# A bias table's relu tiles spread over VectorE, GpSimd and ScalarE, with its log table in PSUM and its output copies on two engines

## The chip, the core and the metric

One core of one Trainium2 chip runs the kernel. Its engines are TensorE (PE, with its weight loads as PEld), VectorE (DVE), ScalarE (ACT), GpSimd (POOL) and SyncE (SP), which here only issues DMAs. The metric is device time in microseconds, the median of several runs. VectorE and ScalarE reach PSUM as well as SBUF; TensorE writes its products to PSUM.

## The reference

```python
def _attn_ref(q, k, v, w1, b1, w2):          # q, k, v: (4, 8, 576, 64); hidden = 32
    scores = scale * np.matmul(q, k.transpose(0, 1, 3, 2))
    rel = (pos[:, None] - pos[None, :]).astype(np.float32)
    psi_rel = np.log1p(np.abs(rel))
    psi_i = np.log1p(np.maximum(pos[:, None].astype(np.float32), 1.0))
    x = (psi_rel / psi_i)[..., None]
    h = np.maximum(x @ w1 + b1, 0.0)
    bias = h @ w2                             # (576, 576, 8): one table for all batches
    scores = scores + bias.transpose(2, 0, 1)[None, :, :, :]
    attn = softmax(scores)
    return np.matmul(attn, v)

# layer 1: x = max(x@w1, x@w2, x@w3) @ w_out      # 2304 tokens, 512 -> 768 -> 512
# layer 2: out = g(x @ w_in) @ w_out                         # 512 -> 2048 -> 512
```

## The kernel before

The kernel has four stages one after the other: the bias table, attention (32 pairs of batch and head), and the two feed-forward layers. Each engine runs its own list of instructions in order and waits on semaphores for the others. The change touches the first stage only.

**The bias table.** `log_t` [128, 1148] holds log(1 + |n|) for every distance n, shifted per partition: partition p = 32 r + c belongs to row r of a group of four query rows and to hidden unit c. `row_sc` holds, per partition and group, w1 divided by the log of the query position. A *group* is four rows (G4 = 4), a *super-tile* (here: a bias tile) is four groups or 16 rows, and NSUP = 36 bias tiles make 576 rows. They are worked on in rounds of four: i is the round (0 to 8), j or e the place in it (0 to 3).

For bias tile s four relu tiles [128, 576] are made, g = 0 to 3: each is relu(log_t shifted by s and g, times row_sc, plus b1). g = 0 to 2 are made by VectorE (`hidden`, line 768) as max(x * row_sc, -b1), which is the relu less b1; g = 3 by ScalarE (`hidden_act`, line 571). The constant that is missing is computed once (`nconst`, line 585) and added at the copy. The relu tiles lie in `hid[e]`, four buffers in the memory of xT. TensorE multiplies each by `w2b` (`bias_tile`, line 941): 8 matmul calls, 16 instructions, into the two PSUM banks 2e and 2e+1, so four bias tiles fill the eight banks. ScalarE copies the two banks to `bias_o[:, e]` in SBUF (`bias_copy`, line 578), and SyncE stores it to `bias_scratch` in DRAM (`store_bias`, line 371).

**The waits.** A relu tile waits until the bias tile four before it has been multiplied (`bias_ps`). `bias_tile` waits for its relu tiles (`hid_ok`, `hid_act`) and for the copy of the bias tile four before (`bias_sb`). A copy waits for its bias tile and for `bias_free[e]`, which the store of four tiles before raises; for the first four it is raised by SyncE itself (line 367) after it has issued the loads of q, k and v for the first two heads (lines 330 to 352). On ScalarE the order is relu s, copy s-2, relu s+1, copy s-1 and so on.

**Around it.** GpSimd makes the initial tables and zeroes, then two `dup`s of q and k (line 493), and then waits for attention. SyncE loads the first head's bias back from DRAM in pieces (`load_first_bias`, line 376): 864 KB after the stores of round 6 are issued, 144 KB after those of round 7, the rest once all stores have landed, followed by line 396 (its tail) and by the second head's bias. TensorE's first transposes of attention (line 968) wait for all copies, since they use the same banks. The first step of attention on VectorE (line 811) waits for the first head's bias.

## Time and profile before

| | |
|---|---|
| time, median of 3 runs | 1166.76 us (1163.58 to 1167.42) |
| span of the profiled execution | 1165.9 us |
| what lies around the span, against the median | 0.9 us |
| TensorE busy | 1110.3 us, 95% |
| VectorE busy | 661.2 us, 57% |
| ScalarE busy | 592.9 us, 51% |
| GpSimd busy | 323.9 us, 28% |
| bias table: first relu to end of last copy | 6.4 to 63.3 us |

The page gives busy time over the whole span. The stages have different limits, so the stage of a change has to be read by itself, from the start and end of single instructions. An instruction's duration may overlap the next one's on the same engine, so the distance from start to start (the pitch) is given where it counts. Times in rows are microseconds from the start of the span, unless marked ns.

### The profile page before, as it was taken

The numbers are of one execution on the slowest core, as the hardware profiler recorded it, in microseconds if no ns is written. First come the engines' busy times: TensorE is split into PE (matmuls) and PEld (weight loads), VectorE is DVE, ScalarE is ACT, GpSimd is POOL, SyncE is SP. The second block draws the span as 40 slices with busy tenths as digits, with TensorE's granted clock in tenths as the row PEclk, the third lists the DMA queues.
The fourth block names the chain that finished last, engine by engine and source line by source line (L and its number), as shares of the span: only waits on it lengthen the run. The fifth ranks groups of instructions, "written<-read, shape, count | busy, mean of one in ns | idle before, by whom it ended". The sixth has DMA issues, their size and how long they took to land.

```text
span 1165.9 us, 21224 instructions
## 1 busy us (share of the span) xinstructions
PE 1110.3 (95%) x6872; PEld 1013.0 (87%) x6872; DVE 661.2 (57%) x1441; ACT 592.9 (51%) x1226; POOL 323.9 (28%) x463
## 2 busy tenths in 40 slices
PE   6878999999999989999999999799999999999998
PEld 2358999999999979999999999777898998989997
DVE  8958888888888952323132222577544444444443
ACT  7957888888888863312121121344434344343433
POOL 4026767767767745300000000344000000000000
PEclk9979999999999999999999999899999999999999
DMA  3651141141141014200000000132000000000000
GB/s 133 215 176 36 42 132 41 41 132 41 41 132 41 21 36 144 74 1 1 0 0 0 0 0 1 55 109 91 28 1 27 0 0 27 0 27 0 28 1 28
DMA packets 68197, 55.29 MB, mean 47 GB/s; under 512 B 28224, under 2 KB 53824, under 8 KB 68160
## 3 DMA queue, kind: packets, MB, share of 16 engines
q1 hardware_dynamic: 68160, 54.81, 15.1%
q8 instruction: 21, 0.34, 0.1%
q14 instruction: 16, 0.13, 0.0%
HBM read 39.46 MB, written 15.34 MB: 47 GB/s over the span
## 4 chain that ended last, share of the span: by engine, by line
PE 80%; DVE 6%; ACT 3%; issue 3%; POOL 0%; ACTq 0%; DVEq 0%
PE ps L1088 34%; PE ps L1133 15%; PE ps L981 11%; PE ps L1036 6%; PE ps L1100 6%; PE ps L1048 5%; DVE tb L906 3%; ACT w_hi L664 1%; DVE s_sb L811 1%; PE ps L968 1%; PE ps L1064 1%; ACT tb L726 1%; PE ps L1072 1%; DVE x_lo L853 1%; ACT ta L720 1%
## 5 line engine op out<-in xcount | busy, mean ns | idle before, releaser
L1088 PE MATMUL ps<-x_hi,w_hi 128*128 128x384 f32 x816 | 277.5, 340 | 16.1 <-POOL w_lo L552 5.8
L1088 PE MATMUL ps<-x_hi,w_lo 128*128 128x384 f32 x816 | 275.5, 338 | 0.0
L1088 PE MATMUL ps<-x_lo,w_hi 128*128 128x384 f32 x816 | 275.3, 337 | 0.0
L1088 PEld LDWEIGHTS ps<-x_hi,w_hi 128*128 128x128 f32 x816 | 154.8, 190 | 26.8 <-POOL w_lo L552 11.8
L1088 PEld LDWEIGHTS ps<-x_lo,w_hi 128*128 128x128 f32 x816 | 154.8, 190 | 3.3
L552 POOL TENSOR_TENSOR w_lo<-raw,w_hi 128x1024 fp32r<-128x1024 f32 x27 | 64.9, 2407 | 324.4 <-ACT w_hi L664 324.2
L1088 PEld LDWEIGHTS ps<-x_hi,w_lo 128*128 128x128 f32 x816 | 154.6, 189 | 0.0
L811 DVE CUSTOM_DVE_ANT_0 s_sb<-ps,bias_h 128x576 f32<-128x576 f32 (+1 forms) x160 | 120.3, 752 | 40.7 <-PE ps L1036 30.4
L502 POOL TENSOR_SCALAR probs<-probs,row_inv 128x512 f32<-128x512 f32 (+1 forms) x160 | 108.4, 693 | 103.4 <-DVE row_inv L785 103.4
L623 ACT ACTIVATE probs<-s_sb,row_min 128x576 f32<-128x576 f32 (+1 forms) x160 | 124.3, 777 | 15.0 <-DVE row_min L811 11.5
L604 ACT ACTIVATE p_hi<-ps 128x512 fp32r<-128x512 f32 (+1 forms) x160 | 88.9, 556 | 52.7 <-PE ps L1048 37.5
L1133 PE MATMUL ps<-w_hi,g_lo 128*128 128x512 f32 x288 | 114.0, 396 | 0.0
L1133 PE MATMUL ps<-w_lo,g_hi 128*128 128x512 f32 x288 | 113.7, 395 | 0.0
L1133 PE MATMUL ps<-w_hi,g_hi 128*128 128x512 f32 x288 | 112.4, 390 | 0.0
L720 ACT ACTIVATE ta<-ps 128x384 f32<-128x384 f32 x96 | 47.0, 489 | 118.1 <-PE ps L1088 117.5
L795 DVE TENSOR_TENSOR p_lo<-ps,p_hi 128x512 fp32r<-128x512 f32 (+1 forms) x160 | 101.3, 634 | 9.9 <-ACT p_hi L604 4.6
L1048 PE MATMUL ps<-ident,probs 128*128 128x128 f32 (+1 forms) x640 | 104.3, 286 | 1.0 <-DVE p_lo L795 1.0
L867 DVE TENSOR_TENSOR tb<-ps,ta 128x384 f32<-128x384 f32 x36 | 20.1, 558 | 144.6 <-PE ps L1088 144.6
L906 DVE TENSOR_TENSOR tb<-tb,tc 128x384 f32<-128x384 f32 x96 | 79.1, 823 | 37.6 <-ACT tb L726 37.6
L1048 PEld LDWEIGHTS ps<-ident,probs 128*128 128x128 f32 (+1 forms) x640 | 91.8, 206 | 8.1 <-issue 7.9
L900 DVE TENSOR_SCALAR tb<-ta 128x384 f32<-128x384 f32 x96 | 34.6, 360 | 113.1 <-ACT ta L720 110.9
L730 ACT ACTIVATE g_hi<-tb 128x384 fp32r<-128x384 f32 x96 | 50.4, 525 | 94.8 <-DVE tb L906 94.8
(105 smaller groups left out, 2110.1 us busy)
## 6 DMA issues: line engine op xcount, KB each, us to landing
bias_scratch<-probs SPq DMA_DIRECT2D x36, 288.0 KB, 2.1
bias_h<-bias_scratch SPq DMA_DIRECT2D x7, 1152.0 KB, 5.7
raw<-in_moe_w_out SPq DMA_DIRECT2D x22, 256.0 KB, 3.1
raw<-in_moe_w SPq DMA_DIRECT2D x18, 256.0 KB, 3.2
out<-o_sb SPq DMA_DIRECT2D x18, 256.0 KB, 2.1
q_in<-in_q SPq DMA_DIRECT2D x32, 128.0 KB, 2.0
k_in<-in_k SPq DMA_DIRECT2D x32, 128.0 KB, 2.3
v_in<-in_v SPq DMA_DIRECT2D x32, 128.0 KB, 2.5
```

The source lines that it names most:

```text
L502: pool.tensor_scalar(pr, pr, row_inv[0:rows[t], par, t:t + 1], 1.0, ALU.mult, ALU.mult).then_inc(p_norm, 1)
L604: last = act.activation(dst, src, ACT.Copy, scale=scale)
L623: act.activation(probs[0:n, par, t, :], s_sb[0:n, (par + t) % 2, :], ACT.Exp, scale=-1.0, bias=row_min[0:n, par, t:t + 1], accum_out=row_s ...
L795: last = dve.tensor_tensor(dst, src, hi.bitcast(F32), ALU.subtract)
L811: dve.tensor_tensor_reduce(halves(s_sb[0:n, (par + t) % 2, :]), score_ps()[0:n], halves(bias_h[0:n, par, t, :]), 1.0, 3.0e38, ALU.add, ALU ...
L906: dve.tensor_tensor(tb[:, :], tb[:, :], tc[:, :], ALU.add).then_inc(d_g, 1)
L981: last = pe.matmul(ps[:, bank, 0:cols.stop - cols.start], vx[:, at:at + 2, :].rearrange("p a d -> p (a d)"), tx[:, cols] if h is None else ...
L1036: last = pe.matmul(score_ps()[0:n, c, :], q_s[:, par, t * P:t * P + n], kx[:, par, c * HC:(c + 1) * HC], start=(part == 0), stop=(part == 1))
L1048: last = pe.transpose(ps[:, bank, c * n:(c + 1) * n], interleaved(pr[:, 0:MAIN])[:, c, :], ident[0:n, 0:n])
L1088: last = pe.matmul(ps[:, bank, 0:BLK], w[:, at:at + P], x[:, kt, :], start=(kt == 0 and n == 0), stop=(kt == KT - 1 and n == 2))
L1100: last = pe.matmul(ps[:, Y_BANK + dt, 0:BLK], w[:, at:at + P], g[:, ft % 2, :], start=(opens and i == 0), stop=(closes and i == 2))
L1133: last = pe.matmul(ps[:, O_BANK + t, :], g[:, ft % 4, t * P:(t + 1) * P], w[:, wout_d(ft):wout_d(ft) + DM], start=(opens and i == 0), stop ...
```

## The change

VectorE first copies `log_t` to `log_p` in PSUM banks 5 to 7 and makes its relu tiles from there. In each round of four bias tiles with four relu tiles each, VectorE makes 5 (g = 0 of every bias tile and g = 1 of the first), GpSimd 7 (g = 2 of the first, g = 1 and 2 of the others) and ScalarE 4 (g = 3 of all). GpSimd reads `log_t` in SBUF; it makes its first seven tiles ahead of the two `dup`s. Bias tiles use PSUM banks 0 to 3 only: even ones banks 0 and 1, copied by ScalarE, odd ones banks 2 and 3, copied by VectorE with a tensor_scalar. So a bias tile waits for the copy of the one two before it. The copies stand in new places of the two engines' orders: VectorE, round i: relus of (i,0), copy (i-1,3), relu of (i,1), relu of (i,2), copy (i,1), relu of (i,3); ScalarE: copy (i-1,2), relus of (i,0) and (i,1), copy (i,0), relus of (i,2) and (i,3). `hid` keeps its four buffers, the stores their order.

```diff
--- before.py
+++ after.py
@@ -128,6 +128,15 @@
             o_sb = sb("o_sb", [P, 3, DM], c=moe)
         ps = ctx.enter_context(nc.psum_tensor("ps", [P, 8, 512], F32))
+        log_p = ps[:, 5:8, :].rearrange("p b n -> p (b n)")
+        HID_DVE = ((0, 1), (0,), (0,), (0,))
+        HID_POOL = ((2,), (1, 2), (1, 2), (1, 2))
+        HID_ACT = 3
+        def hid_done(share, i, j):
+            return i * sum(len(g) for g in share) + sum(len(g) for g in share[:j + 1])
         O_SPLIT = 2 * P
@@ -146,10 +155,10 @@
         a_rows = sem("a_rows")
         const_ps = sem("const_ps")
         const_sb = sem("const_sb")
-        hid_ok = sem("hid_ok")
-        hid_act = sem("hid_act")
+        log_ps = sem("log_ps")
+        hid_dve, hid_pool, hid_act = sem("hid_dve"), sem("hid_pool"), sem("hid_act")
         bias_ps = sem("bias_ps")
-        bias_sb = sem("bias_sb")
+        bias_sb = [sem(f"bias_sb{e}") for e in range(2)]
         bias_free = [sem(f"bias_free{e}") for e in range(4)]
         bias_in = [sem(f"bias_in{e}") for e in range(2)]
         qk_in = [sem(f"qk_in{e}") for e in range(2)]
@@ -366,10 +375,10 @@
             for e in range(4):
                 sp.sem_inc(bias_free[e], 16)
-            def store_bias(s, e):
-                sp.wait_ge(bias_sb, s + 1)
-                sp.dma_start(bias_d[ds(s * SUP, SUP), :, :].rearrange("i h j -> (i h) j"),
-                             bias_o[:, e, :]).then_inc(bias_free[e], 16)
+            def store_bias(i, j):
+                sp.wait_ge(bias_sb[j % 2], 2 * i + j // 2 + 1)
+                sp.dma_start(bias_d[ds((4 * i + j) * SUP, SUP), :, :].rearrange("i h j -> (i h) j"),
+                             bias_o[:, j, :]).then_inc(bias_free[j], 16)
             def load_first_bias(lanes):
@@ -379,7 +388,7 @@
             with sp.Fori(0, NSUP // 4 - 2) as i:
                 for j in range(4):
-                    store_bias(4 * i + j, j)
+                    store_bias(i, j)
             done = 0
             for left in (2, 1):
@@ -389,7 +398,7 @@
                 load_first_bias(lanes)
                 done = lanes.stop
                 for j in range(4):
-                    store_bias(NSUP - 4 * left + j, j)
+                    store_bias(NSUP // 4 - left, j)
             for e in range(4):
                 sp.wait_ge(bias_free[e], 16 * (NSUP // 4 + 1))
             load_first_bias(slice(done, P))
@@ -538,8 +547,26 @@
                     if par == 1:
                         normalise_tails(1, PART_A)
+            def hidden(i, j, first):
+                for g in HID_POOL[j]:
+                    if not first and g == HID_POOL[j][0]:
+                        pool.wait_ge(bias_ps, 4 * i + j - 3)
+                    s = 4 * i + j
+                    pool.tensor_scalar(hid[j][:, g, :], log_t[:, ds(ZERO_AT - s * SUP - g * G4, S)],
+                                       row_sc[:, ds(s * 4 + g, 1)], nb1[:, 0:1],
+                                       ALU.mult, ALU.max).then_inc(hid_pool, 1)
+            pool.wait_ge(a_dve, 5)
+            pool.wait_ge(a_act, 3)
+            for j in range(4):
+                hidden(0, j, True)
             dup(0, 0)
             dup(1, 1)
+            for i in range(1, NSUP // 4):
+                for j in range(4):
+                    hidden(i, j, False)
             steps(pool, step)
@@ -564,35 +591,38 @@
             act.wait_ge(a_dve, 5)
             act.wait_ge(a_act, 3)
-            def hidden_act(s, e, first):
+            def hidden(i, j, first):
+                s = 4 * i + j
                 if not first:
                     act.wait_ge(bias_ps, s - 3)
-                act.activation(hid[e][:, 3, :], log_t[:, ds(ZERO_AT - s * SUP - 3 * G4, S)], ACT.Relu,
-                               scale=row_sc[:, ds(s * 4 + 3, 1)], bias=b1c[:, 0:1]).then_inc(hid_act, 1)
-            def bias_copy(s, e, free):
-                act.wait_ge(bias_ps, s + 1)
-                act.wait_ge(bias_free[e], 16 * (free + 1))
-                act.activation(halves(bias_o[:, e, :]), ps[:, 2 * e:2 * e + 2, 0:HC], ACT.Identity,
-                               scale=-1.0, bias=nconst[:, 0:1]).then_inc(bias_sb, 1)
-            hidden_act(0, 0, True)
-            hidden_act(1, 1, True)
+                act.activation(hid[j][:, HID_ACT, :], log_t[:, ds(ZERO_AT - s * SUP - HID_ACT * G4, S)], ACT.Relu,
+                               scale=row_sc[:, ds(s * 4 + HID_ACT, 1)], bias=b1c[:, 0:1]).then_inc(hid_act, 1)
+            def bias_copy(i, j):
+                act.wait_ge(bias_ps, 4 * i + j + 1)
+                act.wait_ge(bias_free[j], 16 * (i + 1))
+                act.activation(halves(bias_o[:, j, :]), ps[:, 0:2, 0:HC], ACT.Identity,
+                               scale=-1.0, bias=nconst[:, 0:1]).then_inc(bias_sb[0], 1)
+            hidden(0, 0, True)
+            hidden(0, 1, True)
             act.wait_ge(const_ps, 1)
             act.activation(nconst[0:96, :], ps[0:96, 4, 0:1], ACT.Copy, scale=-1.0).then_inc(const_sb, 1)
             act.wait_ge(const_sb, 1)
-            for s in range(2, 4):
-                hidden_act(s, s, True)
-                bias_copy(s - 2, s - 2, 0)
+            bias_copy(0, 0)
+            hidden(0, 2, True)
+            hidden(0, 3, True)
             with act.Fori(1, NSUP // 4) as i:
-                for j in range(4):
-                    hidden_act(4 * i + j, j, False)
-                    bias_copy(4 * i + j - 2, (j + 2) % 4, i - 1 if j < 2 else i)
-            for s in range(NSUP - 2, NSUP):
-                bias_copy(s, s % 4, NSUP // 4 - 1)
+                bias_copy(i - 1, 2)
+                hidden(i, 0, False)
+                hidden(i, 1, False)
+                bias_copy(i, 0)
+                hidden(i, 2, False)
+                hidden(i, 3, False)
+            bias_copy(NSUP // 4 - 1, 2)
             def step(m, par, i):
                 e = 1 - par
@@ -760,20 +790,40 @@
-            def hidden(s, e, first):
-                for g in range(3):
-                    if not first and g == 0:
+            dve.tensor_copy(log_p[:, 0:LTW], log_t[:, :]).then_inc(log_ps, 1)
+            dve.wait_ge(log_ps, 1)
+            def hidden(i, j, first):
+                s = 4 * i + j
+                for g in HID_DVE[j]:
+                    if not first and g == HID_DVE[j][0]:
                         dve.wait_ge(bias_ps, s - 3)
-                    dve.tensor_scalar(hid[e][:, g, :], log_t[:, ds(ZERO_AT - s * SUP - g * G4, S)],
+                    dve.tensor_scalar(hid[j][:, g, :], log_p[:, ds(ZERO_AT - s * SUP - g * G4, S)],
                                       row_sc[:, ds(s * 4 + g, 1)], nb1[:, 0:1],
-                                      ALU.mult, ALU.max).then_inc(hid_ok, 1)
-            for s in range(4):
-                hidden(s, s, True)
+                                      ALU.mult, ALU.max).then_inc(hid_dve, 1)
+            def bias_copy(i, j):
+                dve.wait_ge(bias_ps, 4 * i + j + 1)
+                dve.wait_ge(bias_free[j], 16 * (i + 1))
+                dve.tensor_scalar(halves(bias_o[:, j, :]), ps[:, 2:4, 0:HC], -1.0, nconst[:, 0:1],
+                                  ALU.mult, ALU.add).then_inc(bias_sb[1], 1)
+            hidden(0, 0, True)
+            hidden(0, 1, True)
+            hidden(0, 2, True)
+            dve.wait_ge(const_sb, 1)
+            bias_copy(0, 1)
+            hidden(0, 3, True)
             with dve.Fori(1, NSUP // 4) as i:
-                for j in range(4):
-                    hidden(4 * i + j, j, False)
+                hidden(i, 0, False)
+                bias_copy(i - 1, 3)
+                hidden(i, 1, False)
+                hidden(i, 2, False)
+                bias_copy(i, 1)
+                hidden(i, 3, False)
+            bias_copy(NSUP // 4 - 1, 3)
             def inverse(m, par, part, tiles):
@@ -928,27 +978,28 @@
                 last = pe.matmul(ps[32 * g:32 * g + 32, 4, 0:1], w2b[:, :], b1c[:, :], start=True, stop=True)
             last.then_inc(const_ps, 1)
-            def bias_tile(s, e, first):
-                pe.wait_ge(hid_ok, 3 * s + 3)
-                pe.wait_ge(hid_act, s + 1)
-                if first and e == 2:
-                    pe.wait_ge(const_sb, 1)
-                if not first:
-                    pe.wait_ge(bias_sb, s - 3)
+            def bias_tile(i, j, first):
+                pe.wait_ge(hid_dve, hid_done(HID_DVE, i, j))
+                pe.wait_ge(hid_pool, hid_done(HID_POOL, i, j))
+                pe.wait_ge(hid_act, 4 * i + j + 1)
+                if not first or j >= 2:
+                    pe.wait_ge(bias_sb[j % 2], 2 * i + j // 2)
                 for c in range(2):
                     for g in range(4):
-                        last = pe.matmul(ps[32 * g:32 * g + 32, 2 * e + c, 0:HC], w2b[:, :],
-                                         hid[e][:, g, c * HC:(c + 1) * HC], start=True, stop=True)
+                        last = pe.matmul(ps[32 * g:32 * g + 32, 2 * (j % 2) + c, 0:HC], w2b[:, :],
+                                         hid[j][:, g, c * HC:(c + 1) * HC], start=True, stop=True)
                 last.then_inc(bias_ps, 1)
-            for s in range(4):
-                bias_tile(s, s, True)
+            for j in range(4):
+                bias_tile(0, j, True)
             with pe.Fori(1, NSUP // 4) as i:
                 for j in range(4):
-                    bias_tile(4 * i + j, j, False)
+                    bias_tile(i, j, False)
             pe.wait_ge(ident_ok, 1)
-            pe.wait_ge(bias_sb, NSUP)
+            for e in range(2):
+                pe.wait_ge(bias_sb[e], NSUP // 2)
+            pe.wait_ge(hid_dve, hid_done(HID_DVE, NSUP // 4 - 1, 3))
             def step(m, par, i):
                 e = 1 - par
```

## Rows read from the trace of the kernel before

**Rows 1.** The page: busy time by engine, then VectorE's busy tenths in 40 slices.

```profile
PE 1110.3 (95%) x6872; PEld 1013.0 (87%) x6872; DVE 661.2 (57%) x1441; ACT 592.9 (51%) x1226; POOL 323.9 (28%) x463
...
DVE  8958888888888952323132222577544444444443
```

**Rows 2.** Groups, 0 to 200 us: busy us, mean ns, idle before.

```profile
L768 DVE TENSOR_SCALAR xT<-log_t,row_sc,nb 128x576 f32 x96 | 48.7, 592 | 0.0
L941 PE MATMUL ps<-xT,w2b 128*32 128x288 f32 x576 | 44.7, 430 | 9.8 <-ACT xT L571 5.2 <-DVE xT L768 3.3 <-ACT probs L578 0.9
...
L578 ACT ACTIVATE probs<-ps,nconst 128x576 f32<-128x576 f32 x36 | 27.3, 762 | 6.2 <-PE ps L941 4.4 <-DMA bias_scratch<-probs 1.7
```

**Rows 3.** Timeline of VectorE, merged (start, length, instruction, count), from 30 us.

```profile
29.52 6.94 DVE L768 TENSOR_SCALAR xT<-log_t,row_sc,nb 128x576 f32 x14
```

**Rows 4.** Timeline of ScalarE, 50 to 52 us.

```profile
50.11 0.93 ACT L571 ACTIVATE xT<-log_t,b1c,row_sc 128x576 f32 x1
50.87 0.80 ACT L578 ACTIVATE probs<-ps,nconst 128x576 f32<-128x576 f32 x1
51.49 0.94 ACT L571 ACTIVATE xT<-log_t,b1c,row_sc 128x576 f32 x1
```

**Rows 5.** Timeline, SyncE's last load and the first copy on ScalarE.

```profile
12.74 0.63 SPq L352 DMA_DIRECT2D v_in<-in_v  x1
...
13.52 0.74 ACT L578 ACTIVATE probs<-ps,nconst 128x576 f32<-128x576 f32 x1 [4.44 <-PE ps L941]
```

**Rows 6.** Timeline, end of the bias table and first step of attention.

```profile
52.52 0.65 SPq L376 DMA_DIRECT2D bias_h<-bias_scratch  x1
...
59.74 0.74 ACT L578 ACTIVATE probs<-ps,nconst 128x576 f32<-128x576 f32 x1 [1.69 <-DMA bias_scratch<-probs]
...
61.13 2.14 ACT L578 ACTIVATE probs<-ps,nconst 128x576 f32<-128x576 f32 x3
...
66.28 0.58 SPq L376 DMA_DIRECT2D bias_h<-bias_scratch  x1
...
70.22 0.76 DVE L811 CUSTOM_DVE_ANT_0 s_sb<-ps,bias_h 128x576 f32<-128x576 f32 x1 [3.03 <-DMA bias_h<-bias_scratch]
```

**Rows 7.** Timeline of TensorE: first three bias tiles (48 instructions), and later ones.

```profile
7.98 5.42 PE L941 MATMUL ps<-xT,w2b 128*32 128x288 f32 x48
...
16.52 1.18 PE L941 MATMUL ps<-xT,w2b 128*32 128x288 f32 x16 [0.19 <-ACT xT L571]
...
19.29 2.49 PE L941 MATMUL ps<-xT,w2b 128*32 128x288 f32 x32 [0.20 <-ACT xT L571]
```

**Rows 8.** VectorE: two lines' durations (min/median/max ns), and timeline rows.

```profile
L917 DVE COPY o_sb<-ps x6: 683/684/691, 830.8 to 1161.3; 128x512 f32<-128x512 f32 x6
L885 DVE COPY xT<-ps x12: 543/550/558, 496.4 to 744.4; 128x384 f32 x8, 128x384 f32<-128x384 f32 x4
...
1143.08 0.36 DVE L900 TENSOR_SCALAR tb<-ta 128x384 f32<-128x384 f32 x1 [1.46 <-ACT ta L720]
...
95.85 0.67 DVE L795 TENSOR_TENSOR p_lo<-ps,p_hi 128x512 fp32r<-128x512 f32 x1
96.44 0.75 DVE L811 CUSTOM_DVE_ANT_0 s_sb<-ps,bias_h 128x576 f32<-128x576 f32 x1
```

**Rows 9.** Timeline of GpSimd: dups, tails and normalise.

```profile
10.12 7.21 POOL L493 TENSOR_SCALAR q_dup<-q_in 128x640 f32<-128x640 f32 x1 [4.55 <-DMA k_in<-in_k]
17.30 0.92 POOL L493 TENSOR_SCALAR k_dup<-k_in 128x640 f32<-128x640 f32 x1
...
84.35 0.72 POOL L493 TENSOR_SCALAR k_dup<-k_in 128x640 f32<-128x640 f32 x1
85.06 1.47 POOL L508 TENSOR_SCALAR p_tail<-probs,row_inv 128x64 f32<-128x64 f32 x5
89.72 2.02 POOL L502 TENSOR_SCALAR probs<-probs,row_inv 128x512 f32<-128x512 f32 x3 [3.19 <-DVE row_inv L785]
```

**Rows 10.** Busy us PE, PEld, DVE, ACT, POOL; granted clock, DMA share, GB/s.

```profile
68.00:70.00 2.00, 1.40 (x7) 0.98 (x5) 0.00 (x0) 0.00 (x0) 0.00 (x0) 0.50 0.97 196
```

## The prediction, made before the changed kernel was built

> **What bounds the kernel now.** The page comes first: TensorE is busy 95% of the span, but VectorE is at eight or nine tenths only in the first slices [rows 1]. The change touches that first stretch alone, the building of the bias table, so this is the stage to read. The groups of the first 200 us show three steady streams there: 108 relu tiles on VectorE, 36 relu tiles and 36 output copies on ScalarE, 36 bias tiles on TensorE [rows 2] (of the relus, 96 stand in the row shown and 12 in one of another form). TensorE needs 1.18 us of a tile and waits after each [rows 7]; it is not the bound.
>
> Merged rows of one engine give the pitch (start to start) behind a duration: (length minus one duration) / (count minus 1). VectorE's relu tiles last 0.575 us but follow each other every (6.94-0.575)/13 = 0.490 us, and keep that pitch from 6.4 to 61 us with no idle time [rows 3]: 1.47 us for the three of a bias tile. ScalarE alternates a relu (0.76 us to the next start) and a copy (0.62), 1.38 us a tile, from 13.5 us on [rows 4]. So ScalarE starts late, runs faster, and meets VectorE at about 54 us. Its late start has nothing to do with TensorE, which the row names: the first copy waits for bias_free, which SyncE raises only after its q, k and v loads, issued until 13.4 us [rows 5]. The change leaves that as it is.
>
> The end is a chain of its own. Number the bias tiles 0 to 35 and the copies with them. Copy 27 starts at 50.87, SyncE issues the 864 KB bias load at 52.52, and the stores behind it land late, so copy 32 stands still until 59.74, 7.2 us after that issue. The last copy ends at 61.13+2.14 = 63.27, the last piece of the first head's load goes out at 66.28, and attention starts on it at 70.22 [rows 6]. Everything later hangs on that: a microsecond on the last copy is a microsecond on the end.
>
> **The change part by part.** (1) Relu tiles on VectorE: 108 to 45, read from PSUM. A copy of 512 elements from PSUM takes 0.684 us and one of 384 takes 0.550, so 1.05 ns an element and 0.15 us fixed [rows 8]. The old relu, SBUF to SBUF, cannot run at that rate (576 would alone be 0.60 us): at half of it, it is 0.30 plus 0.275; constants in place of its two per-partition operands give 0.355 for 384, i.e. 0.20 plus 0.155 [rows 8], so the two operands cost 0.12. A relu from PSUM, which I cost at the rate of the copies, is then 0.60 + 0.275 = 0.875 us. The next start is 0.085 earlier, as now: 0.79. The old one cost 0.49, so each relu gets 0.30 dearer.
>
> (2) VectorE gains 18 copies from PSUM with one such operand: 0.60 + 0.155 + 0.06 = 0.82 us, pitch 0.735. Its work per round of four tiles is 5 x 0.79 + 2 x 0.735 = 5.42 us, against 12 x 0.49 = 5.88. Bounds: p_lo reads PSUM at a pitch of 0.59 for 512 elements [rows 8], which makes 0.66 for 576; without any overlap it is 0.875 and 0.82.
>
> (3) GpSimd: 7 relu tiles a round. normalise, with one per-partition operand, has a pitch of (2.02-0.69)/2 = 0.67 for 512 elements and p_tail one of about 0.29 for 64, so 0.73 for 576; with a second operand I take 0.78, and 0.9 as the upper bound, which is what a dup of 640 took beside VectorE [rows 9]. 7 x 0.78 = 5.5 us a round. GpSimd does its first seven at 6.4, then both dups (4 x 0.72), whose loads are in by 13, and is free at 14.6. Moved behind those seven, the dups cost nothing: their reader is the first transpose, after the last copy. Before, the first dup took 7.21 us, since it and VectorE's tiles kept each other out, and VectorE started only about one tile per dup less [rows 9]; that goes, worth some 1.5 us to VectorE in this stretch.
>
> (4) ScalarE: per round 4 x 0.76 + 2 x 0.62 = 4.3 us instead of 5.5. It will have slack by its work.
>
> (5) The waits, which decide. PSUM holds two bias tiles instead of four, and copies stand between relus on in-order engines. On VectorE, copy (i,1) comes after the relu of (i,1) and only one more relu. From the start of relu (i,1): 0.875 until it is done, 0.05 for the semaphore (the usual gap in these rows), 1.18 for the TensorE tile, 0.05 again: 2.155 us until the copy can start, while VectorE has only 0.79 or 1.58 of work. It stands 0.6 us, and behind it the relus of (i,3) and the next round. The second copy has three relus ahead, 2.37 us, more than 2.155: no wait. Round: 2.155 + 0.735 + 2.37 + 0.735 = 6.0 us. ScalarE has such a chain too: copy, relu, tile, copy: 2 x (0.62 + 0.87 + 0.05 + 1.20 + 0.05) = 5.58 us, so even a VectorE that is twice as fast gives no round under 5.58. Work removed: ScalarE's, which was not what ended last; work added: waiting. TensorE alone would allow 4 x 1.24 = 5.0 (two tiles in 2.49 us [rows 7]).
>
> (6) Start: the copy of the log table is 1148 x 1.05 + 0.15 = 1.35 us, so the first relu starts at 7.75 and tile 0 at 9.45; hidden, as the first copy waits for 13.52 anyway. Then copy 0 to 14.14, relu (0,2) to 15.0, tile 2 15.05 to 16.23, tile 3 16.28 to 17.46, copy 3 at 17.5. The first tiles of before took 5.42/3 = 1.8 us each although the granted clock is given as full [rows 7]; if tile 2 still does, 0.3 to 0.6 more.
>
> (7) Copy 27 is six rounds after copy 3: 17.5 + 6 x 6.0 = 53.5, against 50.87. The 864 KB load goes out 1.65 later, at 55.15, copy 32 can start 7.2 after that, at 62.35 (it would be ready at 60.9, so the store still ends last). Then relu (8,2) to 63.84, tile 34 to 65.1, tile 35 to 66.3 (it cannot run ahead, with two PSUM slots), copy 35 to 67.2. Against 63.27 that is +3.9 us; the DMA queues, loaded a little more thinly, may give back 0 to 0.6; the slow tile may take 0.3. I take **+3.6 us**.
>
> Nothing past 70 us is changed. TensorE's granted clock is at the lower of its two levels, 0.50 or 1.2 GHz, from 68 us [rows 10], after TensorE had waited for that last bias load; the same wait stands there after the change, so the same price, shifted. The profiled execution's span is 1165.9, 0.9 under the median 1166.76; I give the time against the median: 1166.8 + 3.6 = **1170.4 us**.
>
> **A rule against the change.** The copies from PSUM and the relu tiles from SBUF share a fixed part of 0.15 to 0.16 us here [rows 8]. The Trainium skill ("VectorE: DVE Perf Modes", The TRN2 errata) instead gives PSUM-source instructions 62 cycles more of fixed cost than SBUF-source ones, about 0.065 us. By that rule relu and copy would be 0.94 and 0.885, the round about 2.22 + 0.80 + 2.57 + 0.80 = 6.4 us, and copy 27 2.3 us later still. The rows speak against it, so it has part of the chance of rival B.
>
> **Rivals.** A, not slower: the chain is shorter than I make it, because the relu from PSUM has the pitch of p_lo (0.66 to 0.70) and lasts 0.75 to 0.79. VectorE's round is then 2.03 + 0.66 + 2.03 + 0.66 = 5.4 and ScalarE's 5.58 decides: copy 27 at 51.0, last copy at 64.3, **+1 us, 1167.8**. It decides from a relu pitch below 0.70. For it: p_lo's pitch. Against: the operands' 0.12 us in the old relu. 0.20.
>
> B, slower: relu and copy do not overlap (0.875 and 0.82), or GpSimd needs 1.0 us a tile. The first gives a round of 2.155 + 0.82 + 2.63 + 0.82 = 6.4, +6 us; the second 7.0, copy 27 at 59.6, **+11 us**. GpSimd decides from 0.86. 0.14.
>
> C: VectorE still shuts GpSimd out, as in the 7.21 us dup. The two engines then take turns, 7 x 0.73 + 7 x 0.77 = 10.5 us a round, **+40 us**. Against it: normalise keeps its pitch of 0.67 in attention [rows 9], where VectorE mostly reads PSUM [rows 8]. 0.04.
>
> D, faster: waits overlap better than in-order chains allow, TensorE's 1.24 us a tile is the pace, and the stores land in time: tile 27 at 15.05 + 25 x 1.24 = 46.1, last copy at 58, **-5 us, 1161.5**. It would need ScalarE's relu (i,2) ready before its copy (i,0), against the written order. 0.07.
>
> **How the numbers follow.** A measurement of this kernel can tell about 0.3%, 3.5 us, from no change. The forecast case (+1.5 to +6) has 0.55; two fifths of it lie under +3.5. Same: 0.20 + 0.22 = 0.42. Slower: 0.33 + 0.14 + 0.04 = 0.51. Faster: 0.07. The range leaves out C, D and the far half of B: 1166 to 1176.
>
> **What will show it.** Relu tiles from log_p at 0.875 us (A: 0.75; B: no overlap); VectorE idle about 0.6 us before every copy (i,1) and none before (i,3); GpSimd's relu near 0.78; bias tiles of TensorE 1.5 us apart on average; copy 27 near 53.5, the 864 KB load near 55.2, the last load near 70. It is wrong if VectorE never waits in the loop (then the order costs nothing), if GpSimd is busy without a gap, or if the last copy ends before 63.

## The result and the profile after

The change made the kernel much slower: 1257.13 us median (1253.91 to 1258.62) against 1167.09 (1163.58 to 1167.44), a ratio of 1.078 with a 95% interval of 1.075 to 1.080. That is +90 us, where +3.6 was forecast and 1176 us was the upper end of the range. The profiled execution took 1253.91 us, with a span of 1252.1.

The page of the changed kernel, busy time and slices:

```profile
PE 1137.1 (91%) x6872; PEld 1015.1 (81%) x6872; DVE 657.3 (52%) x1397; ACT 582.5 (47%) x1208; POOL 459.3 (37%) x526
...
DVE  4333278888888888433222132257744445444443
ACT  3222278888888888542112121134533434343433
POOL 9999856767767676460000000034400000000000
PEclk9955579999999999999999999989999999999999
```

VectorE's first slices, at eight and nine tenths before [rows 1], are now at two to four, and ScalarE's, at seven and nine before, at two and three; that stretch lasts five slices instead of two. GpSimd is the engine that is full there. The groups of that stage (0 to 180 us; busy us, mean ns, idle before) say why:

```profile
L556 POOL TENSOR_SCALAR xT<-log_t,row_sc,nb 128x576 f32<-128x576 f32 x63 | 142.7, 2277 | 0.7 <-DVE row_sc L787 0.7
L990 PE MATMUL ps<-xT,w2b 128*32 128x288 f32 x576 | 74.4, 663 | 71.8 <-POOL xT L556 36.8 <-ACT xT L599 28.7 <-issue 4.1
L802 DVE TENSOR_SCALAR xT<-ps,row_sc,nb 128x576 f32 x40 | 32.8, 867 | 0.0
L810 DVE TENSOR_SCALAR probs<-ps,nconst 128x576 f32<-128x576 f32 x18 | 14.7, 817 | 97.3 <-PE ps L990 97.3
L606 ACT ACTIVATE probs<-ps,nconst 128x576 f32<-128x576 f32 x18 | 13.3, 740 | 103.3 <-PE ps L990 97.8 <-SPq L376 5.5
```

A relu tile takes GpSimd 2.27 us, and it makes 63 of them. It idles 0.7 us before them in all, at the very start, and everyone else waits: VectorE 97 us before its copies, ScalarE 103. The end of the stage, timeline rows:

```profile
151.90 2.15 PE L990 MATMUL ps<-xT,w2b 128*32 128x288 f32 x16 [2.40 <-POOL xT L556]
154.11 0.82 DVE L810 TENSOR_SCALAR probs<-ps,nconst 128x576 f32<-128x576 f32 x1 [7.35 <-PE ps L990]
...
161.31 0.76 DVE L861 CUSTOM_DVE_ANT_0 s_sb<-ps,bias_h 128x576 f32<-128x576 f32 x1 [1.54 <-PE ps L1087]
```

The last copy ends at 154.93 instead of 63.27, +91.7 us; attention's first step on VectorE starts at 161.31 instead of 70.22 [rows 6], +91.1; the medians differ by 90. So the difference lies in this stage, and it can be added up from one row: 6.2 (start) + 63 x 2.27 + 2.8 (the two pairs of dups) = 152.0, then one bias tile and one copy. (The two profiled spans differ by 86.2 only. From its first to its last step on VectorE attention takes 348.7 us in the profile of before and 344.8 in this one. TensorE's granted clock is at its lower level, 1.2 GHz, for 17.6 us of the first 40 there and for 8.1 here; over the eleven profiles of this case, with the same code in attention, it is 8 to 20 us, and attention takes 344.8 to 348.7.)

### The profile page after: what moved, and what is told of

The parts are those of the page before. It is cut to its first block, busy times and chain, and to the rows that moved or that the text cites. A ratio compares the mean times of both kernels' runs of the same rounds, so it can differ in the third digit from the quotient of the medians.

```text
span 1252.1 us, 21239 instructions
## 1 busy us (share of the span) xinstructions
PE 1137.1 (91%) x6872; PEld 1015.1 (81%) x6872; DVE 657.3 (52%) x1397; ACT 582.5 (47%) x1208; POOL 459.3 (37%) x526
## 4 chain that ended last, share of the span: by engine, by line
PE 74%; DVE 5%; ACT 3%; issue 2%; POOL 0%; ACTq 0%; DVEq 0%
PE ps L1139 32%; PE ps L1184 14%; PE ps L1032 10%; PE ps L1087 6%; PE ps L1151 6%; PE ps L1099 5%; DVE tb L956 3%; ACT w_hi L694 1%; DVE s_sb L861 1%; PE ps L1019 1%; PE ps L1115 1%; ACT tb L756 1%; PE ps L1123 1%; DVE x_lo L903 1%; ACT ta L750 0%
## 5 line engine op out<-in xcount | busy, mean ns | idle before, releaser
L556 POOL TENSOR_SCALAR xT<-log_t,row_sc,nb 128x576 f32<-128x576 f32 x63 | 142.7, 2277 | 0.7 <-DVE row_sc L787 0.7
L990 PE MATMUL ps<-xT,w2b 128*32 128x288 f32 x576 | 74.4, 663 | 71.8 <-POOL xT L556 36.8
L990 PEld LDWEIGHTS ps<-xT,w2b 128*32 128x32 f32 x576 | 23.0, 155 | 122.3 <-issue 66.8
```

Source lines behind the costliest of these rows:

```text
L556: pool.tensor_scalar(hid[j][:, g, :], log_t[:, ds(ZERO_AT - s * SUP - g * G4, S)], row_sc[:, ds(s * 4 + g, 1)], nb1[:, 0:1], ALU.mult, ALU ...
L990: last = pe.matmul(ps[32 * g:32 * g + 32, 2 * (j % 2) + c, 0:HC], w2b[:, :], hid[j][:, g, c * HC:(c + 1) * HC], start=True, stop=True)
```

## Experiments

Times are compared with runs of the kernel before on the same chip. The questions: what makes GpSimd's relu tile take 2.27 us (M: the maximum; P: the second per-partition operand; R: the shifted source; C: another engine in its way)? Is that all of the loss? And was the rest of the prediction's sum right?

### Nine forms of the instruction, one in each round

The edit, with each form drawn together on one line:

```diff
-                    pool.tensor_scalar(dst, src, sc, nb1[:, 0:1], ALU.mult, ALU.max)
+                    if i == 0:   op = pool.tensor_scalar(dst, src, sc, nb1[:, 0:1], ALU.mult, ALU.max)
+                    elif i == 1: op = pool.tensor_scalar(dst, src, sc, 0.0, ALU.mult, ALU.max)
+                    elif i == 2: op = pool.tensor_scalar(dst, src, sc, nb1[:, 0:1], ALU.mult, ALU.mult)
+                    elif i == 3: op = pool.tensor_scalar(dst, src, sc, 1.0, ALU.mult, ALU.mult)
+                    elif i == 4: op = pool.tensor_scalar(dst, src, nb1[:, 0:1], None, ALU.max)
+                    elif i == 5: op = pool.tensor_scalar(dst, src, sc, nb1[:, 0:1], ALU.mult, ALU.add)
+                    elif i == 6: op = pool.tensor_scalar(dst, src, 1.0, 1.0, ALU.mult, ALU.mult)
+                    elif i == 7: op = pool.tensor_scalar(dst, src, 1.0, 0.0, ALU.mult, ALU.max)
+                    else:        op = pool.tensor_scalar(dst, src, sc, nb1[:, 0:1], ALU.mult, ALU.subtract)
```

> Only GpSimd's relu instruction is changed, with another form in each round of seven: round 0 (x*pointer, max pointer) as in the change; 1 (x*pointer, max constant 0); 2 (x*pointer, times pointer); 3 (x*pointer, times constant 1); 4 (max pointer alone); 5 (x*pointer, plus pointer); 6 (times 1, times 1); 7 (times 1, max 0); 8 (x*pointer, minus pointer). So most relu tiles are not the reference's, and only the durations count. Theory M, maximum is a slow operation on GpSimd: rounds 0, 1, 4 and 7 near 2.27 us (4 perhaps shorter), the others 0.73 to 0.82. Theory P, the second per-partition operand is what costs: rounds 0, 2, 5 and 8 near 2.27, rounds 1, 3, 4, 6 and 7 at 0.73 to 0.8. Theory R, the shifted read of the log table from SBUF (or its length) costs: all nine near 2.27. Theory C, VectorE or ScalarE keeps GpSimd from its port: all near 2.27 while those run, and shorter in their idle time.

GpSimd's groups of that kernel, which ran once and is read for its durations only. Rounds 0 to 8 are lines 560, 562, 564, 566, 568, 570, 572, 574 and 576:

```profile
L576 POOL TENSOR_SCALAR xT<-log_t,row_sc,nb 128x576 f32<-128x576 f32 x7 | 15.9, 2298 | 0.0
L560 POOL TENSOR_SCALAR xT<-log_t,row_sc,nb 128x576 f32<-128x576 f32 x7 | 15.9, 2287 | 0.7 <-DVE row_sc L806 0.7
L562 POOL TENSOR_SCALAR xT<-log_t,row_sc 128x576 f32<-128x576 f32 x7 | 15.3, 2223 | 0.0
L574 POOL TENSOR_SCALAR xT<-log_t 128x576 f32<-128x576 f32 x7 | 14.7, 2138 | 0.3 <-PE ps L1009 0.3
L568 POOL TENSOR_SCALAR xT<-log_t,nb 128x576 f32<-128x576 f32 x7 | 11.9, 1726 | 0.1
L564 POOL TENSOR_SCALAR xT<-log_t,row_sc,nb 128x576 f32<-128x576 f32 x7 | 5.7, 852 | 0.0
L570 POOL TENSOR_SCALAR xT<-log_t,row_sc,nb 128x576 f32<-128x576 f32 x7 | 5.7, 839 | 0.0
L566 POOL TENSOR_SCALAR xT<-log_t,row_sc 128x576 f32<-128x576 f32 x7 | 5.1, 755 | 0.4 <-PE ps L1009 0.4
L572 POOL TENSOR_SCALAR xT<-log_t 128x576 f32<-128x576 f32 x7 | 4.5, 686 | 0.2 <-PE ps L1009 0.2
```

Same shape, same shifted source, same neighbours: with two multiplications, or a multiplication and an addition, 0.81 us of busy time each (5.7 / 7); with a maximum behind the multiplication 2.1 to 2.3. P falls: a per-partition operand costs about 0.08 us (0.65, 0.73, 0.81 for none, one, two). R falls, and so does C. M holds for the maximum, but the control in round 8 was slow as well: a subtraction behind the multiplication takes 2.27 us. So it isn't the maximum alone.

### Nine more forms

> As the first kernel of forms, only GpSimd's relu instruction differs, by round: 0 (x*pointer, minimum pointer), 1 (x*pointer, minus 1), 2 (minus pointer alone), 3 (plus pointer alone), 4 (times pointer alone), 5 (minimum pointer alone), 6 (max 0 alone), 7 (x*pointer, is_ge pointer), 8 (plus pointer, times pointer). Most relu tiles are not the reference's; only the durations count. Theory S, a few operations (maximum, and by the last run subtract) are slow whatever stands beside them, each adding about 1.0 to 1.5 us for 576 elements: 0, 1, 2, 5, 6 and 7 at 1.6 to 2.3 us, 3, 4 and 8 at 0.7 to 0.85. Theory F, only mult and add have a fast path and any pair that is not made of them alone falls to a general path of 2.1 to 2.3 us: 0, 1 and 7 near 2.2, single operations other than mult and add near 1.7, as the single maximum was. The two differ in round 1 and 2: if minus is a cheap operation in itself, subtract alone is near 0.75.

The edit is as before, with the nine forms that the expectation lists; this kernel too ran once. Rounds 0 to 8 are again lines 560 to 576:

```profile
L574 POOL TENSOR_SCALAR xT<-log_t,row_sc,nb 128x576 f32<-128x576 f32 x7 | 15.9, 2277 | 0.0
L560 POOL TENSOR_SCALAR xT<-log_t,row_sc,nb 128x576 f32<-128x576 f32 x7 | 15.9, 2281 | 0.7 <-DVE row_sc L806 0.7
L562 POOL TENSOR_SCALAR xT<-log_t,row_sc 128x576 f32<-128x576 f32 x7 | 15.3, 2209 | 0.0
L564 POOL TENSOR_SCALAR xT<-log_t,nb 128x576 f32<-128x576 f32 x7 | 11.9, 1724 | 0.0
L566 POOL TENSOR_SCALAR xT<-log_t,nb 128x576 f32<-128x576 f32 x7 | 11.9, 1723 | 0.0
L568 POOL TENSOR_SCALAR xT<-log_t,row_sc 128x576 f32<-128x576 f32 x7 | 11.9, 1723 | 0.0
L570 POOL TENSOR_SCALAR xT<-log_t,nb 128x576 f32<-128x576 f32 x7 | 11.9, 1718 | 0.0
L572 POOL TENSOR_SCALAR xT<-log_t 128x576 f32<-128x576 f32 x7 | 11.3, 1640 | 0.0
L576 POOL TENSOR_SCALAR xT<-log_t,row_sc,nb 128x576 f32<-128x576 f32 x7 | 5.6, 812 | 0.0
```

Both theories missed. Minimum, is_ge and a subtracted constant behind a multiplication are slow (2.2 to 2.3), which is F's side; but a lone addition (L566) and a lone multiplication (L568) are slow too, at the same 1.72 us as a lone minimum or subtraction. What the 18 forms show is narrower than either theory: two operations, each of them a multiplication or an addition (two additions were not tried), run at 0.65 to 0.81 us; every single operation takes 1.6 to 1.7; every pair with another operation in it 2.1 to 2.3. A reading that fits all 18 is one quick path for "multiply or add, twice" and a slower general one; why it is so is not shown.

### A multiplication instead of the maximum on GpSimd

```diff
-                                       ALU.mult, ALU.max).then_inc(hid_pool, 1)
+                                       ALU.mult, ALU.mult).then_inc(hid_pool, 1)
```

> The changed kernel with maximum replaced by a second multiplication in GpSimd's relu instruction alone (its relu tiles are then not the reference's). Theory M: GpSimd takes 0.78 us a tile, and what is left is the sum of the prediction: rounds of 6.0 us (5.58 if only ScalarE's chain holds), copy 27 near 53.5, last copy end near 67, time +1 to +4 us against the kernel before (1168 to 1171). Theory P or R: 2.27 us a tile as in the change, +90 us. A rival inside theory M, TensorE stays at its lower clock with 2.15 us a bias tile: rounds near 8, +15 to +20 us.

Measured 1172.51 us against 1165.36, ratio 1.007 (1.005 to 1.010): of the 90 us some 83 go with that one word. What is left is twice the forecast. GpSimd takes 0.82 us a tile, and TensorE's bias tiles take 1.18 from the third on, so the expectation's rival with 2.15 us a tile is out. Timeline rows of the steady state and of the end:

```profile
50.56 0.82 DVE L810 TENSOR_SCALAR probs<-ps,nconst 128x576 f32<-128x576 f32 x1
51.30 1.66 DVE L802 TENSOR_SCALAR xT<-ps,row_sc,nb 128x576 f32 x2
...
52.46 0.67 PEld L990 LDWEIGHTS ps<-xT,w2b 128*32 128x32 f32 x16 [1.04 <-issue]
...
53.84 0.82 DVE L810 TENSOR_SCALAR probs<-ps,nconst 128x576 f32<-128x576 f32 x1 [0.89 <-PE ps L990]
54.57 2.44 DVE L802 TENSOR_SCALAR xT<-ps,row_sc,nb 128x576 f32 x3
...
55.77 1.18 PE L990 MATMUL ps<-xT,w2b 128*32 128x288 f32 x16 [0.86 <-DVE xT L802]
...
57.11 0.82 DVE L810 TENSOR_SCALAR probs<-ps,nconst 128x576 f32<-128x576 f32 x1
...
58.78 0.66 SPq L385 DMA_DIRECT2D bias_h<-bias_scratch  x1
...
66.03 0.74 ACT L606 ACTIVATE probs<-ps,nconst 128x576 f32<-128x576 f32 x1 [2.17 <-DMA bias_scratch<-probs]
...
70.11 0.82 DVE L810 TENSOR_SCALAR probs<-ps,nconst 128x576 f32<-128x576 f32 x1 [1.57 <-PE ps L990]
```

The copy at 57.11 is copy 27, that at 50.56 is copy 23: a round is 6.55 us, not 6.0. The first half of it is the chain that was forecast: VectorE stands 0.89 us before copy (i,1) at 53.84. Its terms: relu (i,1) starts at 51.30 and ends 0.87 later, at 52.17; TensorE's first weight load follows at 52.46, 0.29 us on, where I had put 0.05; the copy starts 1.38 after that, where I had 1.23. So 2.54 instead of 2.155 from relu to copy.

The second half is the same chain, which was not forecast. Relu (i,3) starts at 54.57, its bias tile runs from 55.77 to 56.95, and copy (i,3) starts at 57.11, again 2.54 after the relu. By VectorE's own pitch the three relus would have let it start 3 x 0.79 = 2.37 us after 54.57, at 56.94. The row shows no idle time before it, because the last relu's own duration reaches 57.01.

The step from VectorE to TensorE can be read in the trace of before:

```profile
53.52 7.43 DVE L768 TENSOR_SCALAR xT<-log_t,row_sc,nb 128x576 f32 x15
...
58.23 0.77 PEld L941 LDWEIGHTS ps<-xT,w2b 128*32 128x32 f32 x16 [0.82 <-issue]
```

VectorE's relus end at 60.95 and follow each other every 0.49 us, so the last one of bias tile 33, the seventh from the end, ends at 58.01, and that tile's first weight load comes 0.22 us later. TensorE waits for its semaphores one after the other, and the step shrinks with the number that stands in the code behind the one that comes last: 0.29 to 0.32 with three behind it (VectorE's, here), 0.21 to 0.22 with two (VectorE's before, GpSimd's in the change), mostly 0.12 with one (ScalarE's). The kernel below with four tiles of a round on GpSimd does not fit this, with steps of 0.05 and 0.13 from GpSimd and two behind it, so what makes the step is not shown.

### VectorE's copy one place later

```diff
-            bias_copy(0, 1)
             hidden(0, 3, True)
+            bias_copy(0, 1)
...
-                bias_copy(i, 1)
                 hidden(i, 3, False)
+                bias_copy(i, 1)
```

> The run with the multiplication on GpSimd, and in addition VectorE's copy (i,1) put behind its relu (i,3), so that three relus stand before either copy. GpSimd's relu tiles are not the reference's, as there. If the chain relu (i,1), bias tile (i,1), copy (i,1) made the round of 6.55 us, with 0.87 + 0.3 + 1.2 + 0.15 = 2.5 us against two relus, the wait of 0.9 us before that copy goes and the round falls to the next chain: ScalarE's, 2 x (0.62 + 0.87 + 0.3 + 1.2 + 0.15) = 6.3, so 6.2 to 6.35 us, last copy about 2 us earlier, time -2 us against that run. If ScalarE's chain or GpSimd was the bound already, the round stays at 6.5 to 6.6 and the time within 1 us.

1170.13 us against 1164.28, ratio 1.0033 (1.0014 to 1.0053), where the kernel with the old order had 1.007. The last copy ends at 67.60 instead of 70.93, 3.3 us earlier, where 2 were forecast. VectorE's and ScalarE's copies:

```profile
51.60 0.82 DVE L810 TENSOR_SCALAR probs<-ps,nconst 128x576 f32<-128x576 f32 x1
...
53.24 0.74 ACT L606 ACTIVATE probs<-ps,nconst 128x576 f32<-128x576 f32 x1 [0.69 <-PE ps L990]
53.88 1.61 ACT L599 ACTIVATE xT<-log_t,b1c,row_sc 128x576 f32 x2
54.23 0.82 DVE L810 TENSOR_SCALAR probs<-ps,nconst 128x576 f32<-128x576 f32 x1 [0.17 <-PE ps L990]
54.86 0.65 PEld L990 LDWEIGHTS ps<-xT,w2b 128*32 128x32 f32 x16 [1.33 <-ACT probs L606]
...
56.19 0.74 ACT L606 ACTIVATE probs<-ps,nconst 128x576 f32<-128x576 f32 x1 [0.70 <-PE ps L990]
...
57.51 0.82 DVE L810 TENSOR_SCALAR probs<-ps,nconst 128x576 f32<-128x576 f32 x1
```

The wait shrinks from 0.89 to 0.17 and the round from 6.55 to 5.91 (57.51 - 51.60): the order of VectorE's list had been the bound. Now ScalarE's own chain is, 2.95 us for half a round (56.19 - 53.24): copy 0.64, relu 0.86, 0.12 to the tile, 1.18, 0.15 to the next copy. I had expected 6.3 for it, since I gave its step to TensorE the 0.3 us that VectorE's has; it takes 0.12. So even with a quick GpSimd and a better order the stage comes back to the 5.88 us a round that VectorE needed before.

### GpSimd's share to VectorE, the rest of the change kept

```diff
-        HID_DVE = ((0, 1), (0,), (0,), (0,))
-        HID_POOL = ((2,), (1, 2), (1, 2), (1, 2))
+        HID_DVE = ((0, 1, 2), (0, 1, 2), (0, 1, 2), (0, 1, 2))
+        HID_POOL = ((), (), (), ())
...
-                    dve.tensor_scalar(hid[j][:, g, :], log_p[:, ds(...)], ...)
+                    dve.tensor_scalar(hid[j][:, g, :], log_t[:, ds(...)], ...)
...
-                pe.wait_ge(hid_pool, hid_done(HID_POOL, i, j))
```

> The changed kernel with GpSimd's seven relu tiles of a round made by VectorE, and all twelve of VectorE read from the table in SBUF; two PSUM slots and the copies by turns stay as in the change. If GpSimd alone cost the 90 us, this loses only what VectorE's extra work costs: 12 x 0.49 + 2 x 0.735 = 7.35 us a round plus a wait of about 0.4 for bias tile (i,1), so 7.4 to 7.8 against 5.9 before, last copy near 80, +14 to +18 us. If the two PSUM slots or the copies by turns are at fault too, the round comes out over 10 us and the time over +40.

1183.13 us against 1165.36, ratio 1.016 (1.013 to 1.018), +17.8 us, as expected. VectorE's relu tiles have their 0.575 us again, and a round is 7.85 us (copies at 50.14 and 57.99). The two PSUM slots and the copies on VectorE cost that at most; they don't make 90 us.

### Four tiles of a round on GpSimd instead of seven

```diff
-        HID_DVE = ((0, 1), (0,), (0,), (0,))
-        HID_POOL = ((2,), (1, 2), (1, 2), (1, 2))
+        HID_DVE = ((0, 1), (0, 1), (0, 1), (0, 1))
+        HID_POOL = ((2,), (2,), (2,), (2,))
```

> The changed kernel with four relu tiles of a round on GpSimd instead of seven, and eight on VectorE, from PSUM. If the maximum on GpSimd is the whole loss, the stage follows its count: 6.2 + 36 x 2.27 + 2.9 (the dups) = 90.8 for GpSimd's last tile, rounds of 9.1 us, last copy near 94, against 154.9 in the change and 63.3 before: +28 to +32 us on the kernel before. VectorE has 8 x 0.79 + 2 x 0.735 = 7.8 us a round and waits inside. If those waits came on top (VectorE's chain in line with GpSimd's), the round would be over 10 us and the time over +40.

1194.83 us against 1164.39, ratio 1.026 (1.020 to 1.033), +30.4 us. The relu line of GpSimd (min/median/max ns, first and last start):

```profile
L556 POOL TENSOR_SCALAR xT<-log_t,row_sc,nb x36: 2272/2273/2284, 6.3 to 88.4; 128x576 f32<-128x576 f32 x36
```

The last one ends at 90.7, with 90.8 forecast from the count. The loss follows the number of GpSimd's tiles; VectorE's waits fit in beside them.

### The table in SBUF for VectorE, with the slow and with the quick GpSimd tile

```diff
-                    dve.tensor_scalar(hid[j][:, g, :], log_p[:, ds(...)], ...)
+                    dve.tensor_scalar(hid[j][:, g, :], log_t[:, ds(...)], ...)
```

> The changed kernel with VectorE's five relu tiles of a round read from the table in SBUF instead of its copy in PSUM. If VectorE's SBUF to SBUF tensor_scalar and GpSimd's exclude each other, each of the five waits out a GpSimd tile or holds one up: 7 x 2.27 + 5 x 0.5 = 18.4 us a round instead of 15.9, +20 to +25 us against the change, and VectorE rows of 2 us and more. If they don't, the round stays 15.9, since GpSimd is the bound, and the time stays within 2 us of the change.

1262.11 us against 1165.36, ratio 1.084 (1.081 to 1.086), where the change has 1.078: 5 to 7 us slower than the change, not 20 to 25. VectorE's relu tiles, by their line, and GpSimd's:

```profile
L802 DVE TENSOR_SCALAR xT<-log_t,row_sc,nb x45: 566/910/1086, 7.6 to 149.5; 128x576 f32 x40, 128x576 f32<-128x576 f32 x5
...
L556 POOL TENSOR_SCALAR xT<-log_t,row_sc,nb x63: 2278/2285/2485, 6.3 to 153.0; 128x576 f32<-128x576 f32 x63
```

VectorE's median is 0.91 us instead of 0.575; none of its rows reaches 2 us. GpSimd's tile does not hold it off for its whole length, and loses little itself: 3.6 us over 63 tiles. Attention's first step starts just that much later, at 164.9 instead of 161.3. The rest lies behind the stage, where the code is the same: attention takes 348.5 us in this profile, with 17.3 us of its start at the lower clock, and 344.8 in that of the change, with 8.1.

With the quick tile (the multiplication kept):

> The run with the multiplication on GpSimd (its relu tiles are not the reference's), and VectorE's relu tiles read from the table in SBUF. Theory: VectorE's SBUF to SBUF tensor_scalar and a GpSimd instruction exclude each other for as long as GpSimd's instruction streams, so a fast GpSimd tile is stopped more than the slow one was. Then the two take turns: 7 x 0.81 + 5 x 0.5 = 8.2 us a round at most, with rows of VectorE or GpSimd well over their own length, and the time +5 to +15 us against the run with the table in PSUM. If the table's place makes no difference, VectorE gains 5 x 0.3 us a round and the round falls from 6.55 to about 6.2.

```profile
L556 POOL TENSOR_SCALAR xT<-log_t,row_sc,nb x63: 814/1017/1152, 6.3 to 68.3; 128x576 f32<-128x576 f32 x63
...
L802 DVE TENSOR_SCALAR xT<-log_t,row_sc,nb x45: 565/1045/1133, 7.6 to 69.3; 128x576 f32 x40, 128x576 f32<-128x576 f32 x5
```

Here both engines pay: GpSimd 1.02 us instead of 0.82, VectorE 1.05 where it needs 0.575 alone. VectorE's relu from SBUF is then no quicker than the 0.87 us from PSUM, the round is 6.7 us (copies at 52.08 and 58.78), and the time, 1172.64 against 1164.28, is that of the table in PSUM within what can be told. The forecast of +5 to +15 was too high: the tiles lengthen each other, but do not add up to turns of full length. So the move of the table to PSUM does cure something that is there, and gains nothing, because its price per relu is the same.

### The kernel before, with an earlier first copy and later dups

```diff
+            for e in range(4):
+                sp.sem_inc(bias_free[e], 16)
             load_qk(0, 0, 0, True)
...
+            pool.wait_ge(hid_ok, 3 * NSUP)
             dup(0, 0)
             dup(1, 1)
```

> The kernel before, with two changes: SyncE raises bias_free before its q, k and v loads instead of after them, so ScalarE's first copy needn't wait until 13.5 us; and GpSimd makes its first two dups after VectorE's last relu tile, so they don't stop VectorE. By the rows VectorE's 108 relus then end at 6.4 + 108 x 0.49 = 59.3 instead of 60.95, copy 27 comes at about 49 instead of 50.9, and the last copy ends near 61.5 instead of 63.3: -1.5 to -2 us. A rival: the pieces of the bias load and their landing set the end, and nothing moves (within 0.5 us).

1163.51 us against 1164.28, ratio 0.9992 (0.9977 to 1.0007): no difference that could be told. In the profiled execution attention's first step does start earlier, at 68.03 instead of 70.22, and the last copy ends at 61.42, with 61.5 forecast, but the time doesn't show the 2.2 us. They aren't given back later in that execution, where attention takes 345.8 us against 348.7 in before's (12.7 us at the lower clock against 17.6). The interval reaches from -2.7 to +0.8 us, so the runs, which spread over 5 us, neither show the forecast gain of 1.5 to 2 us nor rule it out. The two edits were made together, and which of them moved the start isn't shown. It is the only kernel here that is not slower than the one before.

## Why the prediction was wrong

**The step that failed** is (3), GpSimd's relu at 0.78 us with 0.9 as its upper bound. Measured: 2.27, and 7 x 2.27 = 15.9 us a round against 5.5. I took the price of normalise, which has the same instruction name and type, and corrected it for length and operands; those corrections were right (0.81 for two multiplications with two operands, 0.78 forecast). But the operation inside differed, a maximum for a multiplication, and no row of GpSimd in the trace of before had a maximum. All of its TENSOR_SCALAR rows there are two multiplications: the source gives even normalise and the dups, which need one or none, 1.0 as a further factor (by the second kernel of forms a lone multiplication would have taken 1.72 us). So no row named TENSOR_SCALAR could give a warning. The bound should have come from a row with another operation, and there was one. Timeline of GpSimd in the kernel before:

```profile
92.58 0.94 POOL L520 TENSOR_SCALAR v_hi<-v_in 128x896 fp32r<-128x896 f32 x1
93.60 2.11 POOL L523 TENSOR_TENSOR v_lo<-v_in,v_hi 128x896 fp32r<-128x896 f32 x1
```

The subtraction takes 2.11 us, the multiplication of the same size 0.94. I left it aside as an instruction with two inputs. Scaled to 576 elements it gives 1.36 us, past rival B's own point of 0.86, and a GpSimd-bound round of 9.5 us: not the 2.27 us that came, but the right mechanism and some 30 us. Rival B named the mechanism, and stopped at 1.0 us and +11 (by its own rounds of 7.0 us, copy 27 at 59.5 and +10). Of the signs that the prediction gave of being wrong, "GpSimd is busy without a gap" is the one that came.

**(1) and (2), VectorE from PSUM**: 0.875 and 0.82 forecast, 0.868 and 0.817 measured. The fixed part for a PSUM source is that of an SBUF source here; the 0.94 and 0.885 us, estimates worked out from the Trainium skill ("VectorE: DVE Perf Modes", The TRN2 errata), are not seen. Rival A's 0.75 isn't either.

**(4), (6)**: the dups behind the first seven tiles cost only their 2.8 us, which with a GpSimd that is the bound do count. The first copies were as forecast where GpSimd was quick: copy 3 at 17.61, with 17.5 forecast.

**(5), the chains**: shown by the two runs with a quick GpSimd. The wait before copy (i,1) and ScalarE's chain as the next bound were right. The size was not: 6.55 us a round instead of 6.0. Each step from engine to engine stood in the sum as 0.05, "the usual gap in these rows"; from VectorE's relu to TensorE it is 0.29 (0.22 before), from TensorE's tile to the copy about 0.16, from ScalarE's relu to TensorE mostly 0.12. So the chain takes 2.54 us instead of 2.155, which also makes it longer than the three relus (2.37): copy (i,3) waits for its tile too, where no wait was forecast. The round is 2 x (2.54 + 0.735) = 6.55. Six rounds of that make 3.3 us more, and copy 27 came at 57.11 instead of 53.5.

**(7), the tail**: copy 32 at 58.78 + 7.25, with 7.2 forecast; last copy 13.8 us after copy 27, with 13.7 forecast. Had GpSimd been as quick as I took it, the kernel would have come out at about +7 to +8 us, twice my figure and still within the range.

**C** did not happen in the change: GpSimd's tiles take 2.271 to 2.284 us, all alike, whatever VectorE does beside them, and 0.82 with the multiplication. The two engines do slow each other when VectorE goes from SBUF to SBUF, but not by turns of full length. **D** needed rounds of 5.0; none of the kernels with copies by turns came under 5.9.

## What to carry to other kernels

A price goes by the operation inside an instruction, not only by its name, type and size. Before work is moved to GpSimd, find a row with that very operation there (look in the source which one a row stands for), or time it alone; a bound for it must come from the slowest kind of instruction that the trace has on that engine. When copies and the work that feeds them share an in-order engine, count the way from the feeding instruction round to its copy, with the measured gap at each hand-over, and put at least that much other work between them.

## What the runs showed of the hardware that was not expected

- GpSimd's tensor_scalar of [128, 576] in fp32: 0.65 to 0.81 us with two operations out of multiply and add (not both add, which was not tried), 1.6 to 1.7 us with a single operation of any kind tried (also a lone multiplication), 2.1 to 2.3 us with maximum, minimum, subtract or is_ge as the second. Each per-partition operand costs 0.08 us.
- A VectorE relu beside GpSimd's tiles, SBUF to SBUF, takes 0.91 to 1.05 us instead of 0.575, not GpSimd's whole tile, whereas one dup of before stood for 7.21 us beside VectorE's unbroken row of relus [rows 9].
- In the changed kernel most bias tiles take TensorE 2.15 us instead of 1.18, and it waits about 2.4 us before most of them:

```profile
50.00:60.00 10.00, 5.24 (x40) 1.71 (x44) 4.05 (x6) 2.25 (x3) 10.00 (x5) 1.00 0.15 59
...
77.30:80.60 3.30, 1.15 (x16) 0.50 (x16) 0.06 (x1) 2.15 (x3) 3.30 (x2) 1.00 0.30 117
80.70:107.90 27.20, 14.18 (x108) 4.50 (x112) 9.97 (x13) 6.75 (x9) 27.20 (x13) 0.50 0.17 65
```

  The first of the last three columns is the granted clock: 1.00 is its upper level, 2.4 GHz, and 0.50 its lower, 1.2 GHz. The tile that starts at 79.45, in a stretch at the upper level, takes 1.18 us; the next, at 83.96 and at the lower level, 2.15. All tiles of the change that lie wholly within a recorded stretch of either level agree with this. Before 60 us they take 2.15 us although the view gives 1.00, but the trace's first record of the clock stands at 60.19 us, and the tile then running gets quicker (1.70 us): the 1.00 before the first record is no measurement, and the pace is that of the lower level. The same holds for the first tiles of before [rows 7], which the prediction noted as slow at a full clock: the first record there is at 12.70 us, the first two tiles take 2.15 us, and from 15 us on they take 1.18. In before TensorE waits only 0.1 to 0.3 us before most tiles and stays at the upper level until 67 us; in the change, with its waits of 2.4 us, it is there for 13.7 us in all, in four stretches. Each of them begins at the end of two bias tiles that stand 0.1 us apart, but three other such pairs bring none. With four tiles a round on GpSimd, and waits of 1.0 to 1.2 us, it is at the upper level from 26.7 to 94.9 us. The lower clock costs nothing in this stage but one tile at the end, since GpSimd is the bound.
